# One kernel, four small moves near its start: the first pair's k and q in two transfers, and four places in the written order

## What is computed

```python
# factor = 4; scores = scale * q k^T; everywhere: softmax over the last axis
q_d, k_d, v_d = means of 4 neighbouring positions          # 144 pooled positions
out_up    = repeat(softmax(q_d k_d^T) v_d, 4)              # "pooled"
out_local = softmax(where(|i - j| < 4, q k^T, -1e9)) v     # "local"
x = (out_up + out_local) as (2304, 512)
h = max(x @ w1, x @ w2, x @ w3)                            # 512 -> 768
y = h @ w_out                                              # 768 -> 512
z = y @ w_in;  g = max(0.01 z, z);  out = g @ w_out2       # 512 -> 2048 -> 512
```

## Time and profile before

| what | value |
|---|---|
| median of 3 runs | 772.4 us |
| the profiled execution | 771.94 us |
| its span, first to last instruction | 770.2 us |
| granted TensorE clock, mean | 1.000 |
| TensorE matmul busy | 762.8 us, 99% |
| VectorE, ScalarE, GpSimd busy | 446.5, 296.3, 167.0 us |
| chain that ended last | PE 95%, DVE 2%, ACT 1%, DMA 1%, issue 1% |

### The profile page before, as it was taken

The page is one execution under the profiler, slowest core; times in us unless marked ns, Lnnn a source line. Parts: engine busy times, 40 slices in busy tenths (PEclk is TensorE's granted clock), DMA queues, the critical chain, the costliest instruction groups (busy, mean ns, idle before and its releaser), DMA issues.

```text
span 770.2 us, 13539 instructions
## 1 busy us (share of the span) xinstructions
PE 762.8 (99%) x5412; PEld 684.7 (89%) x5412; DVE 446.5 (58%) x769; ACT 296.3 (38%) x697; POOL 167.0 (22%) x208
## 2 busy tenths in 40 slices
PE   9999999999999999999999999999999999999998
PEld 7889989888888889999998988989898998889896
DVE  6867797666745463765756566564434466334433
ACT  4675544333242323433544354442222244222222
POOL 3795121211111333340435533110000000000000
PEclk9999999999999999999999999999999999999999
DMA  8642432332121023212567644446432236223402
GB/s 286 212 161 96 138 119 80 103 96 71 49 76 37 1 68 120 66 44 85 169 254 262 257 178 151 191 152 215 158 118 96 96 133 236 96 97 107 156 25 83
DMA packets 37630, 98.91 MB, mean 128 GB/s; under 512 B 2880, under 2 KB 23360, under 8 KB 34496
## 3 DMA queue, kind: packets, MB, share of 16 engines
q1 hardware_dynamic: 37568, 98.05, 36.4%
HBM read 73.92 MB, written 24.12 MB: 127 GB/s over the span
## 4 chain that ended last, share of the span: by engine, by line
PE 95%; DVE 2%; ACT 1%; issue 1%; DMA 1%; SPq 0%; DVEq 0%; ACTq 0%
PE mlp_ps L1067 10%; PE mlp_ps L1069 9%; PE mlp_ps L1068 9%; PE mlp_ps L1219 8%; PE mlp_ps L1221 8%; PE mlp_ps L1220 8%; PE att_ps L1240 6%; PE att_ps L1242 6%; PE att_ps L1241 6%; PE mlp_ps L1242 3%; PE mlp_ps L1241 3%; PE mlp_ps L1240 3%; PE att_ps L1139 2%; PE att_ps L1141 2%; PE att_ps L1140 2%; PE att_ps L1056 2%
## 5 line engine op out<-in xcount | busy, mean ns | idle before, releaser
L1067 PE MATMUL mlp_ps<-x_hi,wa_lo 128*128 128x288 f32 (+1 forms) x288 | 101.7, 353 | 0.1
L1069 PE MATMUL mlp_ps<-x_hi,wa_hi 128*128 128x288 f32 (+1 forms) x288 | 97.4, 338 | 0.0
L1068 PE MATMUL mlp_ps<-x_lo,wa_hi 128*128 128x288 f32 (+1 forms) x288 | 97.1, 337 | 0.0
L1507 ACT ACTIVATE h_last_a<-wa_raw 128x384 fp32r<-128x384 f32 x72 | 37.8, 524 | 104.7 <-DVE wa_raw L1841 104.1
L1067 PEld LDWEIGHTS mlp_ps<-x_hi,wa_lo 128*128 128x128 f32 x288 | 54.0, 188 | 6.0 <-DVE x_raw L1676 0.3
L1839 DVE TENSOR_TENSOR wa_raw<-mlp_ps,h_raw 128x384 f32<-128x384 f32 x24 | 13.4, 557 | 79.1 <-PE mlp_ps L1221 51.4
L1069 PEld LDWEIGHTS mlp_ps<-x_hi,wa_hi 128*128 128x128 f32 x288 | 54.1, 188 | 4.6
L1068 PEld LDWEIGHTS mlp_ps<-x_lo,wa_hi 128*128 128x128 f32 x288 | 54.3, 188 | 4.0
L1853 DVE TENSOR_TENSOR h_last_b<-wa_raw,h_last_a 128x384 fp32r<-128x384 f32 x72 | 43.3, 605 | 23.5 <-ACT h_last_a L1507 21.1
L855 POOL TENSOR_TENSOR v_rows<-v_rows 72x512 f32<-72x512 f32 x16 | 21.0, 1312 | 152.2 <-DMA v_rows<-in_v_sum 152.2
L1242 PE MATMUL att_ps<-wa_hi,h_last_a 128*128 128x512 f32 x132 | 52.2, 396 | 0.0
(11 more groups left out here) (215 smaller groups left out, 2049.1 us busy)
## 6 DMA issues: line engine op xcount, KB each, us to landing
u_even<-u_scratch SPq DMA_DIRECT2D x8, 1792.0 KB, 7.4
u_odd<-u_scratch SPq DMA_DIRECT2D x8, 1792.0 KB, 7.3
kq_in<-in_kq SPq DMA_DIRECT2D x14, 576.0 KB, 3.9
u_scratch<-u_even SPq DMA_DIRECT2D x4, 1792.0 KB, 8.7
u_scratch<-u_odd SPq DMA_DIRECT2D x4, 1792.0 KB, 9.7
v_rows<-in_v_sum SPq DMA_DIRECT2D x16, 288.0 KB
wa_raw<-in_w SPq DMA_DIRECT2D x6, 768.0 KB, 6.3
v_win<-in_v_band SPq DMA_DIRECT2D x12, 384.0 KB, 3.6
```

Of the source, the lines that this page charges most:

```text
L1067: nc.tensor.matmul(ps, wlo, xhi, start=(n == 0), stop=False)
L1068: nc.tensor.matmul(ps, whi, xlo, start=False, stop=False)
L1069: last = nc.tensor.matmul(ps, whi, xhi, start=False, stop=(n == len(pairs) - 1))
L1507: nc.scalar.activation(g_tile(0, quad, part), g_raw[part], ACT.Copy).then_inc(g_hi_ready, 1)
```

## The change

Five edits, all of which act in the first 42 us or so.

1. Pair 0's k and q come in two transfers: columns 0 to 355 of both, then columns 356 to 575, each with a semaphore of its own. Unit 0's local scores wait for the first alone. Unit 0's sums become two instructions, one over the first part (89 sums each of k and q), one for the 55 remaining sums of k. The pooled scores wait for one sum more than before.
2. Unit 1 computes its pooled scores first, then the local ones.
3. `D 3`, the sums of unit 3, stands ahead of `S 2` instead of behind it.
4. `E 2` stands behind `V 0`, so ScalarE's copy `up` of unit 0 comes ahead of unit 2's exponentials.
5. `N 4` gets due number 2.2 instead of 3.1, `S 5` and `E 5` get 2.3 instead of 2.2, so that unit 4 is normalised ahead of unit 5's scores; `T 4` gets 5.6 instead of 6.0, with the same neighbours as before.

```diff
+KQ_FIRST = -(-(Q_START[2 * PART_MASK[FRONT][1] - 1] + TQ) // FACTOR) * FACTOR     # 356
...
-    put(2.2, ("S", 5), ("E", 5))
+    put(2.3, ("S", 5), ("E", 5))
...
-    return kinds[2:] + kinds[:2] if item[:2] in (("S", 0), ("S", 1)) else kinds
+    return kinds[2:] + kinds[:2] if item[:2] == ("S", 0) else kinds
...
-                sp.dma_start(kq_of(p), kq[divmod(p, PAIRS)]).then_inc(kq_loaded[p % PAIRS], 16)
+                src = kq[divmod(p, PAIRS)]
+                if p == 0:
+
+                    sp.dma_start(kq_of(0)[:, :, 0:KQ_FIRST], src[:, :, 0:KQ_FIRST]).then_inc(kq_first_loaded, 16)
+                    sp.dma_start(kq_of(0)[:, :, KQ_FIRST:S], src[:, :, KQ_FIRST:S]).then_inc(kq_loaded[0], 16)
+                else:
+                    sp.dma_start(kq_of(p), src).then_inc(kq_loaded[p % PAIRS], 16)
...
-                pe.wait_ge(kq_loaded[p % PAIRS], 16 * (p // PAIRS + 1))
+                if u == 0:
+                    pe.wait_ge(kq_first_loaded, 16)
+                else:
+                    pe.wait_ge(kq_loaded[p % PAIRS], 16 * (p // PAIRS + 1))
...
-                pe.wait_ge(sums_ready, u + 1)
+                pe.wait_ge(sums_ready, u + 2)
...
-                if u < 2:
+                if u == 0:
                     local_scores(u)
                     pooled_scores(u)
...
+                if u == 0:
+
+                    done = KQ_FIRST // FACTOR
+                    dve.wait_ge(kq_first_loaded, 16)
+                    nc.vector.tensor_reduce(kq_sum[:, 0, :].rearrange("p (x a) -> p x a", x=2)[:, :, 0:done],
+                                            kq_of(0)[:, :, 0:KQ_FIRST].rearrange("p x (a f) -> p x a f", f=FACTOR),
+                                            AX.X, ALU.add).then_inc(sums_ready, 1)
+                    dve.wait_ge(kq_loaded[0], 16)
+                    nc.vector.tensor_reduce(kq_sum[:, 0, done:SD], kq_of(0)[:, 0, KQ_FIRST:S].rearrange("p (a f) -> p a f", f=FACTOR),
+                                            AX.X, ALU.add).then_inc(sums_ready, 1)
+                    return
```

More of the change, by code:

```diff
@@ L168, in first_phase @@
     put(0, ("LQ", 4))
-    put(2.2, ("S", 5), ("E", 5))
+    put(2.3, ("S", 5), ("E", 5))
     put(1.5, ("LQ", 5))
-    plan = {4: (3.1, 6.0, 7.0, 8.6), 5: (7.6, 9.6, 10.4, 12.0), 6: (11.0, 12.8, 13.8, 15.6), 7: (14.4, 16.4, 20.1, 18.3),
+    plan = {4: (2.2, 5.6, 7.0, 8.6), 5: (7.6, 9.6, 10.4, 12.0), 6: (11.0, 12.8, 13.8, 15.6), 7: (14.4, 16.4, 20.1, 18.3),
             8: (18.5, 21.2, 22.4, 24.2), 9: (22.6, 25.2, 26.2, 28.2), 10: (26.2, 29.5, 30.5, 32.5), 11: (31.2, 34.5, 35.5, 37.5),
@@ L438, in build @@
         mlp_ps = [ctx.enter_context(nc.psum_tensor(f"mlp_ps{i}", [P, 512], F32)) for i in range(BANKS)]
+        kq_first_loaded = sem("kq_first_loaded")
         kq_loaded = [sem(f"kq_loaded{i}") for i in range(PAIRS)]
```

## The result

The changed kernel takes 777.7 us (median of 15 runs, 775.5 to 779.8), the kernel before 772.1 in the same session: the ratio is 1.0067, 95% interval 1.0054 to 1.0081. It is slower by 5.6 us; the interval gives 4.2 to 6.3. The forecast of 772.8 was wrong, and its range (771.2 to 773.8) does not hold the time.

The account below looks back on a forecast made before the run. TensorE was taken as the bound, idle some 4 us, only in the first 42 us. Terms 0.0 + 0.28 + 0.14 + 0 gave +0.4 us: 772.4 on the profiled execution, 772.8 on the median; range 771.2 to 773.8.

Parts of the forecast that it names:

- The loads: Pair 0's two transfers at the start: no gain at the end, pair 1 and all queued behind 0.2 us late.
- d: Delay of pair 1's landing from splitting pair 0's transfer: 0.2 us, or 0.5 at most.
- The third rival: Pair 1's load held up 1 us or more by SP's late issue; 1.5 us late gives 774.1; 5%.
- The sum: Whole kernel: 0.0 for loads and unit 1, 0.28 for `up`, 0.14 for slice 1, 0 for unit 4: +0.4 us.
- The clock: Rival: added idle near 20 us drops TensorE to 1.2 GHz, costing 2.5 to 5 us, 775.3 to 777.8; 3%.
- Unit 1's pooled scores first: Start near 9.15 + d; unit 2's pooled scores move from 12.74 to 12.72; with the loads 0.0 us.
- Unit 3's sums: 1.1 us of VectorE work ahead of unit 2's maximum: cost 0, 0.2 us gained for additions nothing waits for next.
- The copy `up`: ScalarE's copy at 16.86 delays the first large product by 0.28 us, and group 3, through slice 1, by 0.14 more.
- Unit 4's normalisation: The 0.76 us wait at 41.39 goes, but group 6 waits for GpSimd's slice 2 instead: gain 0, up to 0.76.
- those 0.2 us: Group 6's bound: GpSimd could be some 0.2 us slower or faster with other VectorE work beside it.

Follow-up runs that it names:

- halves: The kernel before with pair 0 in two transfers of whole rows, k, then q; 775.8 us, ratio 1.0045.
- on_act: The changed kernel with the second part of pair 0 asked for from ScalarE's queue; 774.5 us, ratio 1.0030.
- no_split: The kernel before with edits 2 to 5 only, pair 0 in one transfer; 772.7 us, ratio 0.9995.
- by_rows: The kernel before with pair 0 in two transfers by partitions, 64 and 64; 775.7 us, ratio 1.0058.
- only_unit1: The kernel before with unit 1's pooled scores first, nothing else; 772.0 us, ratio 0.9994.
- v_first: The kernel before with the v rows asked for ahead of pair 1, no transfer split; 775.6 us, ratio 1.0035.
- split_only: The kernel before with edit 1 alone, pair 0 in two transfers and the order of before; 776.7 us, ratio 1.0053.
- late_second: The kernel before with SP held back ahead of pair 1 until two GpSimd mask pieces are made; 775.2 us, ratio 1.0020.

## Why the prediction was wrong, point by point

**The loads: the step that failed.** "Pair 1's two issues end at about 1.8 ... so the issue hides behind them. All that queues behind is as late as pair 1, d = 0.2 us, or 0.5 at most." The third issue was costed as time on SP, and as such it is hidden. What it moves is the request for pair 1, from 0.43 to 1.35 us behind the first, and from 0.9 us on some of the 16 engines run out of work before it reaches them and deliver it some 2 us late. In place of d = 0.2: 2.34 us. SP's issues were longer too, 0.66, 0.59 and 0.60 us where I took 0.40 from the earlier trace rows; that is 0.4 us of the 0.92, but `halves`, with 0.39 to 0.43, loses as much. I had the data share of 1.06 as proof that nothing was spare; it speaks of 4 us, not of what happens at the change from one transfer to the next. The third rival named the right place and the right mechanism, a request that comes "too late to keep the engines full", and I gave it 5%. It was sized at 1.5 us and 774.1; the load was 2.3 us late. The point from which it was to decide, 7.9, is too late as well: `on_act`, with pair 1's sums at 7.38 (and pair 2's at 10.52 for 9.29), is already 2 us slower. The terms beside it came out: the bulk of pair 1 is 0.2 to 0.3 us late, as priced, and nothing is gained, since unit 0's local scores start at 4.90 in both kernels.

**The sum, again.** Pair 1 late: +2.32 us at unit 1's pooled scores (11.52 for 9.20 in `no_split`). Then 0.55 more by the first large product (28.59 less 25.72, less 2.32): pair 2's sums start 3.0 us late, and unit 1's maximum stands behind them on VectorE. Order edits: +0.18 at group 6 (42.33 for 42.15). Together 3.05, and group 6 is 3.08 late; 0.3 us of the 3.4 come behind it, and no row places them. From the profiled execution to the median it is 2.3 us more, which the clock's falls can account for; no trace of a run at the median was kept.

**The clock.** The rival was right in kind and, for the changed kernel, as far as shown wrong in place: not the 1.1 us at 20 us, but idle times in front of unit 1's scores (2.8 to 3.4 us; 2.3 in `by_rows`), which I didn't foresee since I had pair 1 in time. Its own place isn't safe either: `only_unit1` shows a fall at 21.34, after 1.96 us of idle time. Its price is up to 1.7 us a fall (3.41 us at 1.2 GHz), less than the 2.5 to 5 I gave.

**Unit 1's pooled scores first.** Right: they start behind unit 0's exponentials (9.20 in `no_split`; 9.15 forecast), and unit 2's start at 12.30 in `no_split` and 12.33 in `only_unit1` (12.60 in `no_split_no_up`), where I had 12.52 without d. What the earlier exponentials brought VectorE, 0.34 us, was lost again beside GpSimd (last section).

**Unit 3's sums.** Forecast at cost 0; no run has this edit alone, and no wait in the traces points at it. Unit 3's pooled scores do wait for ScalarE, as forecast: 0.77 us, until 17.75 in `no_split` (18.1 forecast with d).

**The copy `up`.** Right at the end, wrong on the way. I let it start at 16.86 from the earlier trace rows; with unit 1 sooner the v products were over by 16.4 (`no_split` 16.41), so ScalarE lost nothing and the first large product came earlier. The weights behind it were late all the same: slice 1 by 0.40 us, group 6 by 0.38. Forecast for group 6: 0.42.

**Unit 4's normalisation.** Right: no wait in front of its transposes, 0.6 us in front of group 6 for GpSimd instead, in the changed kernel and in both kernels without the split. It is a wait turned into another, with 0.2 us of gain where I had 0: from group 3 to group 6 it takes 8.61 us in before and 8.36 to 8.38 in these three, since GpSimd makes two of the last pieces in 1.15 us instead of 1.36. I had named those 0.2 us as a bound.

## What to carry to other kernels

At a kernel's start, count when the second and third transfers are asked for, not only how many bytes move: a cut that frees the first piece by 0.3 us may put off the request for the next by 0.9, and a few late engines of 16 are as bad as all. An idle TensorE of some 3 us there is, in most executions here, paid twice, by itself and by the half clock after it. Behind a removed wait look for the other engine that feeds the same group; here GpSimd's slice took over, and of the 0.76 us of wait that went, 0.2 us reached group 6.

## What the runs showed of the hardware that I had not expected

In the first 6 us, k and q asked for 0.9 us or more behind the first request ended some 2 us late on one to seven of the 16 engines (in `by_rows` and `v_first` it was later on all 16), and in time, with one half late, when asked for within 0.7 us. In the changed kernel 12 or 13 packets instead of 16 were under way at about 4.8 us, and the longest of those that came next took about 1 us instead of 0.2. The Trainium skill, "DMA: Bandwidth & Descriptors", section "Rules for kernel authors", says that two transfers to disjoint partition halves are not worth making, since they serialise on the same engines. Here they do follow one another (all engines by 4.75 and 5.95 us in `by_rows`), but by that alone `by_rows` would have cost little more than the issue; it lost 3.3 us.

SP took 0.56 to 0.66 us for each of its first three issues where pair 0 was cut by columns or by partitions, against 0.36 to 0.45 in `halves` and `v_first`. It isn't the shape of the transfer alone: in the changed kernel and in `by_rows` the third of them is pair 1, whole, and took 0.60 and 0.59.

VectorE's small sum of `row_sum` (128x14) takes 0.17 us in before. Where it starts while GpSimd adds v rows (1.27 us), it ends 0.02 to 0.04 us behind GpSimd's instruction: 12.71 + 0.51 = 13.22 behind 11.92 + 1.27 = 13.19 in `no_split`, 15.39 + 0.80 = 16.19 behind 14.88 + 1.27 = 16.15 in the changed kernel, and likewise in `halves`, `split_only` and `late_second`. The Trainium skill, "SBUF — State Buffer", section "SBUF: two separate sides", says that the two engines share one pair of ports under an exclusive lock, which a VectorE instruction needs only in a two-port mode or with two SBUF inputs, and that the loser waits for the whole instruction. These five traces agree as to the wait; whether this instruction is of that kind no run shows. In `no_split` it ends at 13.22, as it does in before (13.05 + 0.17), though it starts 0.34 us sooner.
